# Attention and two feed-forward blocks in one kernel: pair 2 of heads takes the ordinary buffers, and the first two steps run in another order

## The reference

```python
scores = scale * np.matmul(q_rot, k_rot.transpose(0, 1, 3, 2))     # q_rot = rotate(q), k_rot = rotate(k)
attn = exp(scores - max) / (sum + 1e-09)
x = attn @ v                                                       # [4, 8, 576, 64] -> [2304, 512]
x = (sigmoid(x @ w_gate) * (x @ w_val)) @ w_out                    # 512 -> 1536 -> 512
h = x @ w_in;  solu = h * softmax(h);  out = (layernorm(solu) * g_ln) @ w_out2     # 512 -> 1024 -> 512
```

## Time and profile before

| | |
|---|---|
| device time, median of 3 runs | 920.06 us (917.46 to 923.15) |
| profiled execution, its own time | 920.06 us |
| span of the trace, first to last instruction | 918.3 us |
| busy share PE, DVE, ACT, POOL | 97%, 47%, 37%, 42% |
| mean granted clock of TensorE | 0.995 |

### The profile page before, as it was taken

How to read it: one execution, slowest core, us unless ns; L and a number is a source line. 1 busy time by engine, 2 the same in 40 slices (tenths; PEclk the granted TensorE clock), 3 DMA queues, 4 the chain that set the end, 5 groups by cost and what they waited for, 6 DMA issues and landing times.

```text
span 918.3 us, 17061 instructions
## 1 busy us (share of the span) xinstructions
PE 891.1 (97%) x6272; PEld 711.0 (77%) x6272; DVE 433.0 (47%) x771; ACT 340.4 (37%) x743; POOL 385.0 (42%) x246
## 2 busy tenths in 40 slices
PE   8799999999899999999999999999999999999998
PEld 6466666666678898888888888888888888888886
DVE  5577777777723333242432243234434654444441
ACT  4688888888721111111111111111111443333332
...
DMA packets 35253, 60.33 MB, mean 66 GB/s; under 512 B 8464, under 2 KB 18192, under 8 KB 35216
## 3 DMA queue, kind: packets, MB, share of 16 engines
...
...
## 4 chain that ended last, share of the span: by engine, by line
PE 77%; POOL 15%; issue 6%; DMA 1%; DVE 1%; SPq 1%; ACT 0%; POOLq 0%; DVEq 0%; ACTq 0%
PE ps L1218 32%; PE ps L1252 16%; PE ps L1318 11%; PE ps L1290 11%; POOL raw_k L667 4%; POOL q_lo L688 2%; POOL raw_q L667 2%; POOL rot_q L672 2%; POOL k_lo L688 2%; POOL x_lo L708 2%; PE ps L1150 2%; PE ps L1199 2%; PE ps L1302 1%; PE ps L1111 1%; PE ps L1178 1%
## 5 line engine op out<-in xcount | busy, mean ns | idle before, releaser
L1218 PE MATMUL ps<-x_hi,w_hi 128*128 128x512 f32 (+1 forms) x480 | 177.0, 369 | 0.0
L1218 PE MATMUL ps<-x_lo,w_hi 128*128 128x512 f32 (+1 forms) x480 | 176.7, 368 | 0.0
L1218 PE MATMUL ps<-x_hi,w_lo 128*128 128x512 f32 (+1 forms) x480 | 176.6, 368 | 0.0
L1039 DVE TENSOR_TENSOR hid<-ps,sig 128x512 f32<-128x512 f32 (+1 forms) x60 | 38.3, 638 | 241.6 <-PE ps L1218 210.0
L873 ACT ACTIVATE sig<-ps 128x512 f32<-128x512 f32 (+1 forms) x60 | 33.3, 555 | 304.6 <-PE ps L1218 304.6
L736 POOL TENSOR_SCALAR w_hi<-raw_w 128x1024 fp32r<-128x1024 f32 x15 | 41.3, 2775 | 215.5 <-PE ps L1252 215.4
L956 DVE TENSOR_REDUCE nmax<-ps 128x1 f32<-128x576 f32 x144 | 108.6, 755 | 38.5 <-PE ps L1150 37.7
L1218 PEld LDWEIGHTS ps<-x_hi,w_hi 128*128 128x128 f32 x480 | 90.5, 189 | 15.7 <-issue 0.9
L833 ACT ACTIVATE prob<-ps,nmax 128x576 f32<-128x576 f32 x128 | 94.8, 741 | 20.9 <-DVE nmax L956 14.9
L1218 PEld LDWEIGHTS ps<-x_hi,w_lo 128*128 128x128 f32 x480 | 90.5, 189 | 15.2
L1218 PEld LDWEIGHTS ps<-x_lo,w_hi 128*128 128x128 f32 x480 | 90.5, 189 | 14.7
...
## 6 DMA issues: line engine op xcount, KB each, us to landing
raw_q<-in_q SPq DMA_DIRECT2D x15, 640.0 KB, 5.0
raw_k<-in_k SPq DMA_DIRECT2D x15, 640.0 KB, 4.4
...
```

What stands on the lines that cost most here:

```text
L1218: last = nc.tensor.matmul(in_parts(gv_ps[f][n][:, 0:size(c)], c), w, x, start=m == 0, stop=m == len(todo) - 1)
```

## The change

Pair 2 is loaded into `raw_q` and `raw_k` like every later pair, so its loads wait for pair 1's products (`FIRST_SP` has `LQ` and `LK` now), and the semaphores `q2_in` and `k2_in` and the wait of DVE in `normal` go. POOL no longer waits for `q0_rot` 3 before it turns pair 1. The copy of q columns 0 to 255 of pair 0 to the upper-left half is a DMA instead of an ACT copy; PE waits for it before `S2`. In step 0 `kB` and `qB` come after `S1` instead of after `S0`. In step 1 POOL takes the loop's order, `qh` comes one tile later and `kh` three items later. `WARM` goes from 17 to 20 pairs; the filler matmuls of step 0 go from 22 to 13 and are spread out.

```diff
-        FIRST_ACT = ["S0", "qB", "S1", "S2", "S3", "S4", "S5", "AB1x", "S6", "AB0x", "S7", "S8", "AB1y"]
-        FIRST_DVE = ["S0", "kB", "qB", "S1", "S2", "S3", "S4", "S5", "S6", "S7", "S8", "AB0y", "INV"]
-        FIRST_SP = ["LV", "T"]
+        FIRST_ACT = ["S0", "S1", "qB", "S2", "S3", "S4", "S5", "AB1x", "S6", "AB0x", "S7", "S8", "AB1y"]
+        FIRST_DVE = ["S0", "S1", "kB", "qB", "S2", "S3", "S4", "S5", "S6", "S7", "S8", "AB0y", "INV"]
+        FIRST_SP = ["LV", "LQ", "T", "LK"]
...
-        SECOND_ACT = ["Qx", "Qy", "S0", "Ky", "S1", "AB2x", "S2", "AB3x", "S3", "qh", "S4", "S5", "S6", "kh", "AB1x", "S7", "AB0x", "S8", "AB1y"]
-        SECOND_POOL = ["ql", "kl", "RQ", "XL", "RK"]
+        SECOND_ACT = ["Qx", "Qy", "S0", "Ky", "S1", "AB2x", "S2", "AB3x", "S3", "S4", "qh", "S5", "S6", "AB1x", "S7", "AB0x", "kh", "S8", "AB1y"]
...
-        WARM = 17
-        FILL = {"S1": 5, "S2": 12, "S3": 1, "S4": 1, "S5": 1, "S6": 1, "S7": 1}
+        WARM = 20
+        FILL = {"S0": 2, "S1": 2, "S2": 2, "S3": 2, "S4": 1, "S5": 1, "S6": 1, "S7": 1, "S8": 1}
...
-                if not early(p, 3):
-                    sp.wait_ge(rotated, 1 if early(p, 4) else num(p) - 1)
+                if not early(p, 2):
+                    sp.wait_ge(rotated, num(p) - 1)
...
+            sp.wait_ge(q0_rot, 2)
+            twice_first(0, slice(0, QM), q0_twice[0])
             sp.wait_ge(q0_rot, 3)
-            twice_first(0, slice(QM, WIDE))
-            twice_first(1, slice(MAIN, WIDE))
-            sp.wait_ge(k0_rot, 2)
-            load(2, q, raw_q0, q2_in, q_rot)
-            load(2, k, raw_k0, k2_in, k_rot)
+            twice_first(0, slice(QM, WIDE), q0_twice[1])
+            twice_first(1, slice(MAIN, WIDE), q0_twice[1])
...
-            pool.wait_ge(q0_rot, 3)
             item("RQ", 1, -1)
...
-            pipeline(pool, ORDER_POOL, item, second=SECOND_POOL)
+            pipeline(pool, ORDER_POOL, item)
...
             for n in range(2):
-                copy_first(1, n * P, n * P + P, n + 1)
-            copy_first(0, 0, QM, 2)
+                copy_first(n * P, n * P + P, n + 1)
...
-                if early(p, 1):
-                    dve.wait_ge(q_rot, 2)
-                    dve.wait_ge(k_rot, 2)
...
-                    if j < 3:
+                    if j < 2:
                         pe.wait_ge(q0_copied, j + 1)
+                    if j == 2:
+                        pe.wait_ge(q0_twice[0], 16)
                     if j == MT:
                         pe.wait_ge(k0_rot, 2)
-                        pe.wait_ge(q0_copied, 4)
+                        pe.wait_ge(q0_copied, 3)
                     if j == MT + 2:
-                        pe.wait_ge(q0_twice, 32)
+                        pe.wait_ge(q0_twice[1], 32)
```

More of the change, by code:

```diff
@@ L215, in build @@
         q_in, k_in = sem("q_in"), sem("k_in")
-        q2_in, k2_in = sem("q2_in"), sem("k2_in")
         v_in = [sem(f"v_in{u}") for u in range(2)]
@@ L229, in build @@
         k0_rot, q0_rot = sem("k0_rot"), sem("q0_rot")
-        q0_copied, q0_twice = sem("q0_copied"), sem("q0_twice")
+        q0_copied, q0_twice = sem("q0_copied"), [sem(f"q0_twice{n}") for n in range(2)]
         k1_rot = sem("k1_rot")
@@ L534, in twice_q, with twice_first @@
                                      ).then_inc(q_twice, 16)
-            def twice_first(r, cols):
+            def twice_first(r, cols, done):
                 sp.dma_start(q_plain[0][ROWS[r], SIDE + cols.start:SIDE + cols.stop], q_plain[0][ROWS[1 - r], cols]
-                             ).then_inc(q0_twice, 16)
+                             ).then_inc(done, 16)
             parts = [w_gate.rearrange("(k p) f -> p k f", p=P), w_val.rearrange("(k p) f -> p k f", p=P)]
@@ L663, in rotate @@
             def rotate(p, raw, arrived, products, prod, lo_done, rot, plain, done):
-                pool.wait_ge(arrived, 16 if early(p, 3) else num(p) * 16 - 16)
-                for dst, tab in products(raw):
+                pool.wait_ge(arrived, num(p) * 16)
+                for dst, tab in products:
                     last = nc.gpsimd.tensor_tensor(dst, dst, tab, ALU.mult)
@@ L673, in rotate @@
                                         ).then_inc(done, 1)
-            def q_products(raw):
-                return [(raw[:, :, 0:MAIN].rearrange("p c (h n) -> p c h n", h=2), twice(tab_q[:, :, 0:QM])),
-                        (raw[:, :, S:], tab_q[:, :, QM:])]
-            def k_products(raw):
-                return [(raw[:, :, TAIL:].rearrange("p c (h n) -> p c h n", h=2), twice(tab_k[:, :, 0:SH])),
-                        (raw[:, :, 0:TAIL], tab_k[:, :, SH:])]
+            q_products = [(raw_q[:, :, 0:MAIN].rearrange("p c (h n) -> p c h n", h=2), twice(tab_q[:, :, 0:QM])),
+                          (raw_q[:, :, S:], tab_q[:, :, QM:])]
+            k_products = [(raw_k[:, :, TAIL:].rearrange("p c (h n) -> p c h n", h=2), twice(tab_k[:, :, 0:SH])),
+                          (raw_k[:, :, 0:TAIL], tab_k[:, :, SH:])]
             def rest(p, piece, rot, hi_done, lo_done):
@@ L691, in item @@
                 if name == "RQ":
-                    rotate(p, *((raw_q0, q2_in) if p == 2 else (raw_q, q_in)), q_products, q_prod, q_lo, rot_q, q_plain, q_rot)
+                    rotate(p, raw_q, q_in, q_products, q_prod, q_lo, rot_q, q_plain, q_rot)
                 elif name == "RK":
-                    rotate(p, *((raw_k0, k2_in) if p == 2 else (raw_k, k_in)), k_products, k_prod, k_lo, rot_k, k_plain, k_rot)
+                    rotate(p, raw_k, k_in, k_products, k_prod, k_lo, rot_k, k_plain, k_rot)
                 elif name == "kl" and not head_first(p):
@@ L847, in turned, with copy_first @@
                 last.then_inc(tr_out[bank], 1)
-            def copy_first(r, a, b, turned):
-                act.wait_ge(q0_rot, turned)
-                nc.scalar.activation(q_plain[0][ROWS[r], SIDE + a:SIDE + b], q_plain[0][ROWS[1 - r], a:b], ACT.Copy).then_inc(q0_copied, 1)
+            def copy_first(a, b, done):
+                act.wait_ge(q0_rot, done)
+                nc.scalar.activation(q_plain[0][ROWS[1], SIDE + a:SIDE + b], q_plain[0][ROWS[0], a:b], ACT.Copy).then_inc(q0_copied, 1)
             def item(name, p, step):
                 if name == "qB":
-                    copy_first(1, QM, MAIN, 3)
+                    copy_first(QM, MAIN, 3)
                 elif name[0] == "S":
```

## The result

In 14 runs of each kernel, alternated on one chip, the changed kernel took 926.44 us in the median (923.35 to 931.42) and the kernel before 920.41 (917.28 to 923.15): the ratio is 1.0077, 95% interval 1.0057 to 1.0095, so 6.0 us slower by the medians, 5 to 9 by the interval. The intervals don't overlap, so one kernel gave two answers; what the profiles show on that follows, and it stays open. The forecast was 923.0 with a range of 918 to 927.

What follows compares the result with a forecast made beforehand. PE, busy 97%, was taken to bound the kernel, so start losses before pair 4 reach the end. +4.3 up to `AB1`, +0.1 in step 1 and -1.5 from stalls gave +2.9 on 920.06: 923.0 us, range 918 to 927.

Steps and rivals of the forecast that it cites:

- The sum: Whole kernel: +4.3 up to `AB1`, +0.1 in step 1, -1.5 from stalls, together +2.9 us, so 923.0.
- What bounds it: PE, busy 97%: time lost or won before pair 4 reaches the end unchanged; loop stays at 14.50 us a pair.
- Warm-up: `S0` at 8.0: Start: three more warm-up pairs take 0.8 us, moving `S0` from 7.21 to 8.0.
- The collision: Step 0: DVE's `kB` and `qB` operations alternate with POOL's from 11.1; `qB` ends at 17.5 (16.2 to 19.1), undisturbed 13.3.
- Rival A: Step 0: no collision, `qB` ends at 13.3, `AB1` 0.4 late, stalls go; -1.0, so 919.1; chance 0.20.
- `qB` to `AB1`, 5.0: Step 0: from `qB`'s end to `AB1` 5.0 us, 3.3 of it from `S4`'s start; `AB1` at 22.5.
- Fillers and the clock, taken as zero: Step 0: half clock may come before `S4` or lift before `S6` to `S8`; zero, bounds -1.2 and +0.8.
- Stalls give back 1.5: Pair 2 to pair 4: PE's waits for POOL's and ACT's late work shrink, 1.5 us back, at most 1.7, at least 0.5.
- The copy by DMA: Step 0: lands about 12.8, free while `qB` ends later; without the collision holds `S2`'s maximum up by 0.3.
- Pair 2's loads: Steps 0 and 1: q lands about 26, k about 28, both turned by 35, needed about 38; hidden, 3 us spare.
- Rival B: Start: POOL wins every time and the clock falls early; +5.8, so 925.9; chance 0.16.

Runs made afterwards that it cites:

- e10: Changed kernel with POOL's wait for `q0_rot` 3 put back and more filler behind `S1`, `S4`, `S5` and `S8`; 918.21 us, ratio 0.9973 to the kernel before.
- e8: Kernel before with more filler in step 0: 3 behind `S4`, 6 behind `S5`, 8 behind `S8`; 918.30 us, ratio 0.9977.
- e9: Kernel before with the pair-2 part of the edit and extra filler behind `S4`, `S5` and `S8`; 917.25 us, ratio 0.9966.
- e1: Changed kernel with one line back, POOL waiting for `q0_rot` 3 before it turns pair 1; 921.26 us, ratio 1.0014 to the kernel before.
- e14: Changed kernel, POOL free, with filler 14 behind `S1`, 12 behind `S3`, 3 behind `S4`, 6 behind `S5`, 8 behind `S8`; 924.44 us, ratio 1.0027 to the kernel before.
- e11: The changed kernel again, unedited, for a second profile, against the kernel before; 924.07 us, ratio 1.0030.
- e4: Kernel before with the changed kernel's `WARM` and `FILL` and nothing else; 921.47 us, ratio 1.0017.
- e2: Kernel before without POOL's wait for `q0_rot` 3 and nothing else; 922.91 us, ratio 1.0013.
- e7: Kernel before with only the pair-2 and hand-over part of the edit, step 0's fillers and POOL's wait kept; 918.94 us, ratio 0.9980.
- e12: Kernel before without POOL's wait for `q0_rot` 3 and with more filler behind `S3`, `S4`, `S5` and `S8`; 919.65 us, ratio 0.9991.
- e5: Changed kernel with 14 fillers behind `S1` and 12 behind `S3` instead of 2 and 2; 924.48 us, ratio 1.0039 to the kernel before.
- e3: Changed kernel with `WARM` and `FILL` of the kernel before; 926.01 us, ratio 1.0057 to the kernel before.
- e6: Changed kernel with the copy of q columns 0 to 255 made by ACT instead of a DMA; 924.02 us, ratio 1.0028 to the kernel before.
- e13: Changed kernel, POOL free, with filler 14 behind `S1`, 20 behind `S3`, 3 behind `S4`, 6 behind `S5`, 8 behind `S8`; 922.14 us, ratio 1.0012 to the kernel before.
- the first comparison: The changed kernel against the kernel before, 14 runs each; 926.44 us against 920.41, ratio 1.0077.
- The second: The changed kernel, unedited, compared with the kernel before once more, 12 runs; 924.07 us against 921.16, ratio 1.0030.

## Why the prediction was right and wrong

*The sum.* In the profiled execution the +6.1 of span is 4.5 up to `AB1`; 1.3 from there to `Q` of pair 0, by the half clock; 1.5 in the late stretch at half clock; and 1.2 given back. Forecast were 4.3, 0, 0, and -1.4 (+0.1 and -1.5). The 4.5 can be divided by e10, where `AB1` comes 6.2 behind the start of `S2` at the copy's landing (20.07 and 13.89). Counted from the landing at 13.16 it would have come at 19.3 without a collision, so the warm-up, the order and the copy make 1.2, the half clock from `S4` on 0.8 (4.49 against 3.71), and the collision 2.6: an estimate. Forecast for these three were 0.1, 0 and 4.2. So the main mechanism, the collision, was right, the sum up to `AB1` came out by errors that cancel, and behind it the sum failed by the clock: 1.3 that the change brings and 1.5 that this execution had besides, with the 0.8 ahead of `AB1` 3.6 in all.

*What bounds it.* Right, to within 1 us. What was lost before pair 4 reached the end: in e8 and e9 pair 4's first tile comes 2.9 and 3.1 earlier than before, and the span is 2.4 and 3.0 shorter; the pace of the loop held (pair 4 to pair 14 in 144.8 us, before 145.0).

*Warm-up: `S0` at 8.0.* 7.72 in one execution and 8.62 in another, the same 40 matmuls taking 6.46 and 7.34. The forecast lies between; that the difference decides something was not seen.

*The collision.* The mechanism, its place and its start were right: POOL at 11.18 by the landing of `raw_q` (forecast 11.1), DVE's operations in turn with POOL's. `qB`'s end was 16.63 and 19.27, forecast 17.5 between 16.2 and 19.1. The Trainium skill, "SBUF — State Buffer", section "Who interferes with whom", calls the port pair that DVE and GpSimd share an exclusive lock. The trace agrees: two DVE products of 0.89 us together take 3.04 to 3.49 beside POOL's. Worked out with each DVE operation behind a whole POOL operation `qB` ended at 19.1 in the prediction, and the full form ends at 19.27. Undisturbed, `qB` ends 5.23 behind `S0`'s start (e1: 8.79 and 14.02), so the collision itself held `qB` up by 2.3 in e14, 3.7 in the profile after and 5.4 in e11, forecast 4.2. Less of it reaches `AB1`, since the copy would have held `S2` up as well: by the estimate above 2.6 and 4.8 in the last two. Rival A, no collision, is refuted by every profile in which the two met. Its price for the rest was too low too: it had `AB1` 0.4 late without a collision, and by e10 it is about 1.2.

*`qB` to `AB1`, 5.0.* Measured 6.1 in both executions: 4.49 instead of 3.3 from `S4` on, 0.8 of it by the half clock (3.71 in e10), 0.4 since I had the chain of exponentials too short. With `qB` ending 0.9 early, `AB1` came at 22.71, forecast 22.5: right by luck, two errors that cancel.

*Fillers and the clock, taken as zero.* This is the step that failed. "The half clock that comes near 18.9 now can come before `S4`" was written, and priced at 0.8 for `S4` and `S5` alone. It came at 11.8, while PE sat idle for the DMA copy, and stayed for 17 us; in e4, with the new filler alone, it came near 12.7 and stayed up to 26. Up to `Q` of pair 0 it cost 1.3 more than the half clock of before, 2.4 more than none (8.94 against 6.58), and it is in the 4.49 too, with 0.8; e4 has +1.2 on each of the two legs. Behind pair 15 another stretch took 1.5; that one comes in profiles of either order (of before's order e2, e7, e8 and e12, not before, e4 and e9; of the changed order the two of the change, e1 and e5, not e3, e6, e10, e13 and e14), so it seems to belong to the execution and not to the change. The bound of +0.8 for the early clock should have been the whole stretch up to pair 1's first tiles: 12 to 29 us.

*Stalls give back 1.5.* Mis-sized. From pair 2's to pair 4's first tile it took 30.54 us against 30.73: 0.2 back (0.9 in e11, 29.84). PE's 0.91 for ACT's copy did go, as forecast, but the wait for `k_lo` at pair 4 grew from 0.56 to 1.16. `RK` of pair 4, named as late next, started at 66.80 and not at 63.3 to 64, since its load landed late. Another 0.7 came back behind pair 4. e7 bears out the direction: without the collision this part of the edit gives 1 to 2.

*The rest.* The copy by DMA landed at 13.1 (forecast 12.8) and costs nothing while a collision holds `qB` up (e6); without one it holds up the maximum of `S2` (by 1.2 in e10), where 0.3 was forecast. Pair 2's loads were hidden. Rival B's figure, 925.9, is near what the first comparison gave, by a milder collision and a dearer clock than it had. The second gave the forecast's 2.9 by its medians, and that is luck too: the profiled execution of that comparison is 7.7 longer than before's, by a full collision and the half clock.
